# Attention with half tiles of keys stacked hi over lo, TensorE waits moved to the matmul that needs each, and new queue orders and PSUM banks

## The reference, cut to what matters

```python
q, k, v: (4, 8, 576, 64)                      # B, H, S, D
q_rot, k_rot = (rotate(q), rotate(k))
scores = scale * np.matmul(q_rot, k_rot.transpose(0, 1, 3, 2))
scores = scores - np.max(scores, axis=-1, keepdims=True)
attn = np.exp(scores)
attn = attn / (np.sum(attn, axis=-1, keepdims=True) + 1e-09)
x = np.matmul(attn, v)                        # to (2304, 512)
h = x @ w_in; r = np.maximum(h, 0.0)          # first MLP, 512 -> 2048 -> 512
x = (s * (r * r) + b) @ w_out
h = x @ w2_in                                 # second MLP, same sizes
out = (h * (1.0 / (1.0 + np.exp(-1.702 * h)))) @ w2_out
```

## Time and profile before

| | us |
|---|---|
| median of 3 runs | 1076.78 (1075.91 to 1077.61) |
| the profiled execution | 1077.13 |
| its span, first to last instruction | 1075.2 |
| outside the span | 1.93 |
| PE busy | 1043.3 (97%) |
| DVE, POOL, ACT busy | 737.1, 706.5, 634.5 |

### The profile page before, as it was taken

One profiled execution on the slowest core, in us unless ns is written; L12 is line 12 of the kernel. 1 busy time (PEld: TensorE's weight loads), 2 busy tenths in 40 slices (PEclk: granted clock), 3 DMA queues, 4 the chain that ended last, 5 costly groups with the idle time before them and its releaser, 6 DMA issues.

```text
span 1075.2 us, 17071 instructions
## 1 busy us (share of the span) xinstructions
PE 1043.3 (97%) x6234; PEld 962.3 (90%) x6234; DVE 737.1 (69%) x874; ACT 634.5 (59%) x1125; POOL 706.5 (66%) x586
## 2 busy tenths in 40 slices
PE   4899999999989999999999999999999999999998
PEld 4799999999988999999999999998888889888887
DVE  6888888889887757755586564875577555854542
ACT  4887878787865545654565454654456434654542
POOL 6878787878888856667556754766566675555420
PEclk9999999999999999999999999999999999999999
DMA  4555455554232221221212221221222422241101
GB/s 107 129 150 150 111 143 143 153 132 114 65 96 71 79 79 59 79 60 59 78 59 80 60 78 60 59 79 59 79 60 69 128 61 78 59 137 59 60 20 59
DMA packets 100613, 93.03 MB, mean 87 GB/s; under 512 B 15652, under 2 KB 78644, under 8 KB 100532
## 3 DMA queue, kind: packets, MB, share of 16 engines
q1 hardware_dynamic: 99408, 90.94, 29.6%
q10 hardware_dynamic: 1124, 1.02, 0.3%
HBM read 69.44 MB, written 4.79 MB: 69 GB/s over the span
## 4 chain that ended last, share of the span: by engine, by line
PE 83%; POOL 5%; DVE 5%; ACT 3%; DMA 2%; issue 1%; SPq 0%; ACTq 0%; POOLq 0%; DVEq 0%
PE psum L1121 37%; PE psum L1093 31%; PE psum L714 6%; PE psum L642 3%; PE psum L668 3%; ACT E L777 2%; DVE negmax L876 1%; DVE Xlo L886 1%; PE psum L744 1%; DVE osum L906 1%; DVE QK L929 1%; POOL win_lo L1038 1%; POOL xT L531 1%; DMA sin<-in_k_sin_dram 0%; POOL osum L527 0%
## 5 line engine op out<-in xcount | busy, mean ns | idle before, releaser
L1038 POOL TENSOR_TENSOR win_lo<-win_raw,win_hi 128x768 fp32r<-128x768 f32 x48 | 101.6, 2116 | 244.2 <-ACT win_hi L1032 244.2
L1093 PE MATMUL psum<-xc_hi,win_hi 128*128 128x384 f32 x672 | 226.7, 337 | 4.2 <-DVE h_b L1299 2.4
L1093 PE MATMUL psum<-xc_lo,win_hi 128*128 128x384 f32 x672 | 226.7, 337 | 0.0
L1093 PE MATMUL psum<-xc_hi,win_lo 128*128 128x384 f32 x672 | 226.1, 336 | 0.0
L1093 PEld LDWEIGHTS psum<-xc_hi,win_hi 128*128 128x128 f32 x672 | 126.8, 189 | 13.7 <-issue 3.8
L1093 PEld LDWEIGHTS psum<-xc_lo,win_hi 128*128 128x128 f32 x672 | 126.7, 189 | 8.2
L1048 POOL TENSOR_TENSOR wout_lo<-wout_raw,wout_hi 128x1024 fp32r<-128x1024 f32 x48 | 119.6, 2492 | 16.5 <-ACT wout_hi L1253 16.5
L1093 PEld LDWEIGHTS psum<-xc_hi,win_lo 128*128 128x128 f32 x672 | 126.8, 189 | 0.0
L777 ACT ACTIVATE E<-psum,negmax 128x576 f32<-128x576 f32 x128 | 94.6, 744 | 13.4 <-DVE negmax L876 13.3
L876 DVE TENSOR_REDUCE negmax<-psum 128x1 f32<-128x576 f32 x128 | 91.0, 751 | 14.1 <-PE psum L642 13.5
L1042 DVE TENSOR_TENSOR win_lo<-wsum,win_hi 128x1024 fp32r<-128x1024 f32 x46 | 95.1, 2068 | 4.2 <-ACT win_hi L1032 4.1
(11 more groups left out here) (154 smaller groups left out, 2852.5 us busy)
## 6 DMA issues: line engine op xcount, KB each, us to landing
wout_raw<-in_moe_w_out_dram SPq DMA_DIRECT2D x48, 512.0 KB, 3.6
win_raw<-in_moe_w_in_dram SPq DMA_DIRECT2D x48, 256.0 KB, 2.8
win_raw<-in_moe_w_in_dram SPq DMA_DIRECT2D x96, 128.0 KB, 2.8
Q<-QK SPq DMA_DIRECT2D x60, 144.0 KB, 2.8
QK<-QK SPq DMA_DIRECT2D x30, 288.0 KB, 3.4
vraw<-in_v_dram SPq DMA_DIRECT2D x32, 128.0 KB, 2.5
raw<-in_q_dram SPq DMA_DIRECT2D x30, 128.0 KB, 2.9
raw<-in_k_dram SPq DMA_DIRECT2D x30, 128.0 KB, 2.7
```

The source lines that it names most:

```text
L1038: pool.tensor_tensor(win_lo[m % 2][:, 0:3 * BLK], win_raw[m % 2][:, 0:3 * BLK], win_hi[m % 2][:, 0:3 * BLK].bitcast(F32), ALU.subtract).th ...
L1093: mm = pe.matmul(hps(n, k), w[n % 2][:, at:at + P], x[k][:, t, :], start=k in FRESH and t == 0 and i == 0, stop=t == HK - 1 and i == 2, sk ...
```

## The change

1. **Stacked half tiles.** `XC[h]` (128 x 640) holds head h's 64 tail keys twice: their hi part in the rows of h, their lo part in the rows of 1 - h. V's tail rows are loaded into both halves. One product per piece then gives hi and lo together. `hiT` and `loT` become two instructions of 64 x 576 each instead of one of 128 x 640. The clearing of `vraw` and SP's wait for it go; a V load has one more transfer.
2. **Waits.** `freed` is called per bank, ahead of the matmul that first writes the bank; X, XT and PV wait per tile.
3. **Orders.** All the order lists and bank lists are new. In the period lists the attention tokens carry an offset that is larger by seven (S@1 is now S@8, PV@-1 is PV@6, V@0 is V@5 and so on), while `program`, `FIRST`, the hooks `after(s)` and the offsets of `H`, `xc`, `wsplit`, `first`, `mid` and `late` are as they were.

```diff
-    PE_ORDER = order("XT@-1 X10@-1 X11@-1 IT@-1 X12@-1 X13@-1 S00@1 PV0@-1 H@-1 S01@1 S02@1 S03@1 ST@1 S10@1 S11@1 "
-                     "S12@1 X00@0 X01@0 S13@1 PV1@-1 prep0@3 X02@0 prep1@3 X03@0 XQ@0")
+    PE_ORDER = order("X03@6 H@-1 XQ@6 X10@6 X11@6 X12@6 X13@6 prep1@9 IT@5 XT@6 S00@8 S01@8 PV0@6 S02@8 S03@8 S10@8 PV1@6 S11@8 "
+                     "X00@7 S12@8 X01@7 S13@8 X02@7 ST@8 prep0@10")
...
-    POOL_ORDER = order("rot1@3 eps@0 V0@0 mid@0 V1@0 vlo0@0 vlo1@0 late@0 finish@-1 rot0@4")
+    POOL_ORDER = order("V0@5 eps@5 vlo0@5 rot1@8 V1@5 mid@0 finish@3 vlo1@5 rot0@9 late@0")
...
-    SLOTS = [1, 0, 5, 7, 1, 4, 3, 1, 2, 0, 1, 3, 0, 2, 1, 7, 6, 0, 2, 1, 7, 2, 1, 6]
+    SLOTS = [6, 5, 4, 2, 3, 1, 3, 0, 2, 1, 0, 3, 1, 0, 3, 2, 0, 7, 1, 6, 2, 7, 0, 1]
...
-            XThi = sb("XThi", [P, S + TAIL], F32R)
-            XTlo = sb("XTlo", [P, S + TAIL], F32R)
+            XC = [sb(f"XC{h}", [P, S + TAIL], F32R) for h in range(2)]
...
-                    sp.dma_start(vraw[rows_of(h), h, NM, :], v_h[2 * p + h, MAIN:S, :]).then_inc(v_in[h], 16)
+                    for half in range(2):
+                        sp.dma_start(vraw[rows_of(half), h, NM, :], v_h[2 * p + h, MAIN:S, :]).then_inc(v_in[h], 16)
...
-                    freed(pe, before[("S", p, h, j)])
                     ps, at = banks("S", p, h, j), (h + j) * P
-                    for a, b, c in PIECES[h]:
+                    for (a, b, c), job in zip(PIECES[h], before[("S", p, h, j)]):
+                        freed(pe, job)
...
+                    for j in range(NM):
+                        pe.wait_ge(et_lo, 2 * NM * p + NM * h + j + 1)
+                        for (a, b, c), job in zip(PIECES[0], before[("PV", p, h, 0)]):
+                            if j == 0:
+                                freed(pe, job)
+                            if h == 0 and j == 0 and b == r + S:
+                                pe.wait_ge(etQ_lo, p + 1)
+                            for n, x in enumerate((Xhi, Xlo)):
+                                pe.matmul(ps[:, a:b], V[h][:, j, :, :].rearrange("p a d -> p (a d)"), x[:, h, j, c:c + b - a],
+                                          start=j == 0 and n == 0, stop=False, skip_group_check=True)
+
+                    pe.wait_ge(etT_lo, 2 * p + h + 1)
+                    for a, b, c in (PIECES[0] if h == 0 else ((r, BANK, TAIL), (BANK, r + MAIN, TAIL + BANK - r), (r + MAIN, r + S, 0))):
+                        mm = pe.matmul(ps[:, a:b], V[h][:, NM, :, :].rearrange("p a d -> p (a d)"), XC[h][:, c:c + b - a],
+                                       start=False, stop=True, skip_group_check=True)
                     mm.then_inc(pv_done, 1)
...
-                def hiT(p, _, __):
+                def hiT(p, h, _):
                     act.wait_ge(xT_t, p + 1)
-                    need(act, pv_done, 2 * p)
-                    act.copy(XThi[:], banks("XT", p)[:, ROW[1]:ROW[0] + S]).then_inc(etT_hi, 1)
+                    need(act, pv_done, 2 * (p - 1) + h + 1)
+                    act.copy(XC[h][rows_of(h), 0:S], row(banks("XT", p), h)[rows_of(h), :]).then_inc(etT_hi, 1)
...
-                def loT(p, _, __):
-                    dve.wait_ge(etT_hi, p + 1)
-                    dve.tensor_tensor(XTlo[:], banks("XT", p)[:, ROW[1]:ROW[0] + S], XThi[:].bitcast(F32), ALU.subtract).then_inc(etT_lo, 1)
+                def loT(p, h, _):
+                    dve.wait_ge(etT_hi, 2 * p + h + 1)
+                    dve.tensor_tensor(XC[h][rows_of(1 - h), 0:S], row(banks("XT", p), h)[rows_of(h), :],
+                                      XC[h][rows_of(h), 0:S].bitcast(F32), ALU.subtract).then_inc(etT_lo, 1)
```

More of the change, by code:

```diff
@@ L89, in fused_kernel @@
-    SLOTS = [1, 0, 5, 7, 1, 4, 3, 1, 2, 0, 1, 3, 0, 2, 1, 7, 6, 0, 2, 1, 7, 2, 1, 6]
-    BANK_ORDER = (6, 0, 7, 1, 2, 3, 4, 5)
-    PE_FIRST = order("prep0@0 prep1@0 S00@0 S01@0 S02@0 prep0@1 S03@0 ST@0 S10@0 prep1@1 X00@0 S11@0 S12@0 S13@0 S00@1 "
[4 rows of a table removed]
-    ACT_FIRST = order("qk0@0 qk1@0 exp00@0 exp01@0 qk0@1 exp02@0 exp03@0 qk1@1 expT@0 hi00@0 exp10@0 exp11@0 exp12@0 "
[5 rows of a table removed]
-    DVE_FIRST = order("klo0@0 klo1@0 max00@0 max01@0 max02@0 klo0@1 max03@0 maxT@0 max10@0 klo1@1 lo00@0 max11@0 "
[5 rows of a table removed]
-    POOL_FIRST = order("rot0@1 rot1@1 rot0@2 rot1@2 V0@0 eps@0 V1@0 vlo0@0 rot0@3 vlo1@0 rot1@3 eps@1 V0@1 vlo0@1 rot0@4 "
-                       "rot1@4 rot0@5 eps@2 V1@1 V0@2 vlo1@1 vlo0@2 rot1@5 finish@0 V1@2 vlo1@2 rot0@6 finish@1")
@@ new lines, in fused_kernel @@
+    ACT_ORDER = order("xc01@-1 xc02@-1 exp02@7 exp03@7 exp10@7 evac1@5 xc03@-1 hi00@6 exp11@7 wsplit@-1 hi01@6 exp12@7 first@-1 "
+                      "exp13@7 hi02@6 qk0@9 hi03@6 hiQ@6 xc04@-1 hi10@6 expT@7 hi11@6 hi12@6 hi13@6 qk1@9 icp@5 hiT0@6 hiT1@6 "
+                      "exp00@8 exp01@8 evac0@6 xc05@-1 xc06@-1")
+    DVE_ORDER = order("max03@7 max10@7 sum1@5 xc01@0 xc02@0 xc03@0 first@0 max11@7 lo00@6 xc04@0 xc05@0 max12@7 xc06@0 max13@7 "
+                      "lo01@6 maxT@7 lo02@6 klo0@9 lo03@6 loQ@6 lo10@6 lo11@6 lo12@6 lo13@6 klo1@9 max00@8 loT0@6 max01@8 loT1@6 "
+                      "sum0@6 inv@6 max02@8")
@@ new lines, in fused_kernel @@
+    POOL_ORDER = order("V0@5 eps@5 vlo0@5 rot1@8 V1@5 mid@0 finish@3 vlo1@5 rot0@9 late@0")
+    SP_ORDER = order("load0@10 kcopy1@8 load1@10 get@4 qcopy0@9 put@5 loadv0@7 loadv1@7 qcopy1@9 kcopy0@9")
+    SLOTS = [6, 5, 4, 2, 3, 1, 3, 0, 2, 1, 0, 3, 1, 0, 3, 2, 0, 7, 1, 6, 2, 7, 0, 1]
+    BANK_ORDER = (6, 0, 7, 1, 2, 3, 4, 5)
+    PE_FIRST = order("prep0@0 prep1@0 S00@0 S01@0 S02@0 ST@0 S03@0 prep0@1 S10@0 X00@0 X01@0 S11@0 S12@0 prep1@1 S13@0 X02@0 X03@0 "
[4 rows of a table added]
+    ACT_FIRST = order("qk0@0 qk1@0 exp00@0 exp01@0 exp02@0 expT@0 exp03@0 qk0@1 hi00@0 exp10@0 hi01@0 exp11@0 qk1@1 exp12@0 hi02@0 "
[4 rows of a table added]
@@ L152, in put @@
             of = banks_of(kind, p, h, j)
-            before[(kind, p, h, j)] = list(dict.fromkeys(last_in[b] for b in of if b in last_in))
+            was = [last_in.get(b) for b in of]
+            before[(kind, p, h, j)] = [job if job not in was[:n] else None for n, job in enumerate(was)]
             for b in of:
@@ L263, in fused_kernel, with freed @@
         x_done = sem("x_done")
-        def freed(eng, jobs):
-            for job in jobs:
+        def freed(eng, job):
+            if job:
                 read(eng, *job)
@@ L279, in read @@
             elif kind == "XT":
[L280 removed]
+                need(eng, etT_lo, 2 * p + 2)
             elif kind == "IT":
@@ L674, in XQ_job @@
                         pe.wait_ge(expT_done, p + 1)
-                    freed(pe, before[("XQ", p, 0, 0)])
+                    freed(pe, before[("XQ", p, 0, 0)][0])
                     ps = banks("XQ", p)
```

83 lines of the change are left out of this document (32 added, 51 removed), and 27 rows, old and new, of tables (ACT_FIRST, DVE_FIRST, PE_FIRST).

## The result

| | before | after |
|---|---|---|
| median, us | 1076.86 (4 runs, 1075.91 to 1077.61) | 1105.26 (4 runs, 1103.36 to 1106.56) |
| ratio, 95% interval | 1 | 1.0263 [1.0248, 1.0277]: slower |
| profiled execution, its span | 1077.13, 1075.2 | 1104.12, 1102.3 |
| PE busy, granted clock | 1043.3, 0.998 | 1040.4, 0.988 |

The forecast was 1092.8 with a range of 1082 to 1099. The direction is right, the size isn't: 12.5 us of the loss were not seen, and the range misses it by 6.

What follows compares the result with a forecast made beforehand. PE was taken to bound attention, busy 17.76 of 18.15 us a period. Periods -2.3, start and last pairs -2.7 and the joint +21.0 summed to +16.0, so 1092.8 us beside the median, range 1082 to 1099.

Steps and rivals of the forecast that it cites:

- The mechanism of the joint: Between attention and MLP: POOL starts window 0's work only after attention's last V; PE stands still some 15 us.
- The waits of the period: In each attention period PE waits in X11 and X13 and before PV0, behind ACT's queue: 1.25 us in all.
- The columns on PE's path: Fewer tail columns in PV0 and PV1 save PE 0.57 us per pair, with bounds of 0 and 0.57.
- The slow clock of the first products: Products (0,0) and (0,1) after the joint run at 1.2 GHz, costing nothing while ACT holds (0,2) back.
- 17.95 us a period: Attention period: 16.7 us of work plus 1.25 of new waits, against 18.15; -2.3 us over eleven periods.
- hidden restarts: PE losses inside "busy" in an attention period, estimated at 0.5 us and taken off the old period.
- Start and last pairs, -2.7: Columns of pairs 0, 13 and 14 give 1.7 us, a new order of the first pairs 1 us.
- the joint, +21.0: Between attention and MLP: product (0,2) starts 32.8 us after PV1 of pair 14 ends, in place of 11.8.
- everything by the same amount: MLP from product (0,2) on: POOL, ACT and DVE keep the old order, so all shifts by +21.0 us.
- hiT and loT in two, no cost: Attention period: second instructions add 0.6 us each to ACT and DVE, both staying below PE.
- the stacked tile gives no time: Rival within the forecast's range: weight loads set the pace, columns of pairs 0, 13 and 14 give nothing; +1.7, 1094.5.
- a worse joint with *no* gain per period: Rival, 15%: low clock from (0,2), POOL slower and further behind, no gain in attention; 1099.3 us.

Runs made afterwards that it cites:

- e11: Changed kernel with everything of the joint moved along with attention (POOL, SP, PE, ACT, DVE, banks) and DVE's `inv` ahead of `xc01`: 1089.66 us.
- e3: Changed kernel with each product of the stacked tail tile issued twice: 1112.82 us, 7.6 above the changed kernel.
- e9: Changed kernel with the joint's labels moved, plus the start lists of the kernel before: 1090.21 us, against 1090.31 with the change's start.
- e2: Changed kernel with the offsets of POOL's period list alone lowered by six: 1102.08 us.
- e1: Changed kernel (stacked half tiles, moved waits) with the queue orders and banks of the kernel before: 1085.48 us, ratio 1.0072 to the kernel before.
- e5: e1 with the half tile of head 1 later, `hiT1` behind `hi11` and `loT1` behind `lo11`: 1108.28 us.
- e10: e1 with PV0 ahead of S00 and the banks changed, so PV0 has those of XQ and IT: 1085.99 us.
- e12: e11 without the stacked tile (128x704 tail tile, two tail products a piece, one hiT and one loT): 1096.05 us.

## Why the prediction was right and wrong

**Right.** The mechanism of the joint: tokens of attention moved by seven, the steps tied to s not, POOL's queue in one row, PE idle for 12 to 18 us (18.2 were measured, just beyond), (0,2) behind ACT. Moving those labels gave 15.6 us back (e11). The waits of the period (X11 for `klo0`, X13 for `expT`, PV0 for `klo1`), each at its place, 0.51 + 0.24 + 0.18 = 0.93, where 1.25 was worked out. The columns on PE's path (e3). The slow clock of the first products: 0.32 us from start to start from 334.85 to 338.05, at 1.2 GHz; they were not the path's end, since (0,2) then waited 0.99 for ACT.

**Right by luck: 17.95 us a period.** Measured were 18.05. Of these 0.93 are waits, so PE's own work is 17.1, where the sum had 16.7: the 0.5 of "hidden restarts" that it took off hardly went. It had been read from two rows (205.60 and 206.75) as the same two jobs, but they are X10, X11 and X12, X13. The work was 0.4 too small and the waits 0.3 too large, and the two errors nearly cancelled.

**The step that failed first: "Start and last pairs, -2.7".** With the period it made t0 5.0 earlier; it came 1.80 later. The period took 1.2 of these 6.8 us (-1.13 over eleven periods, for -2.3). The rest is in this term: -0.94 up to PV1(1), then +0.35 and +3.52 from PV1(12) to PV1(14). I counted the columns and not what the order leaves behind each PV1. The table above shows that between PV1(13) and PV1(14) PE needs 14.1 us in place of 10.6. After a PV1 the new order has S11, S12, S13 and ST of the pair two later and X00 to X02 of the next still to do, at 289.79 to 294.3; the old one has `prep0` and `prep1` there, which the last pairs don't have. The four jobs of scores take 3.4 us from start to start, two waits (for `expT` and for `XC`) take 0.9 in place of 0.2, and the columns give 0.6 back: together the 3.5. In the periods this costs nothing, at the end about 4 us. That is read from the rows; no run changed the order of the last pairs. The gain of 0.94 at PV1(1) is the same thing seen from the other side: e9 with the old start came out the same.

**The second: the joint, +21.0.** From t0 it took 23.9 more (35.7 for 11.8). Of the 2.9 missing, 2.53 is the wait of `finish` for `inv_row`, behind `load_win(1)` on SP. I followed POOL's hooks and not SP's, whose labels had stayed behind in just the same way. e2 shows what they are worth alone: with POOL moved and SP not, POOL waits 11.4 and 9.2 us. `w_sum` took 4.2 for 2.9 and `first_w_hi` 4.2 for 3.3 beside DVE's lo parts of x, 2.2 in place of the 1.5 added for that; ACT's part was the size worked out.

**The third: behind (0,2) "everything by the same amount".** 1.4 us more were lost. PE waits there for `h_a` for 3.0 us, for 1.5 before, and a little behind this wait, from 355.7 on, the products run at the low clock (1.2 GHz), those with `wout` 0.43 us from start to start in place of 0.24:

```profile
354.90 0.45 PE L1094 MATMUL psum<-xc_hi,win_hi 128*128 128x384 f32 x1 [2.96 <-DVE h_a L1143]
```

The kernel before has such a stretch of its own a little earlier, the twelve products behind the wait of 2.35 us, which the changed kernel runs at full clock; over the 25 us from (0,2) on, the granted clock is 0.93 in both. So the low clock takes about the same from both, and what is lost are waits: 5.7 us of them from there on in windows 0 and 1, for 4.1 before. Why `h_a` is late stays open.

Together 6.8 + 2.9 + 1.4 = 11.1, which is 27.1 of span less the 16.0 that were forecast. The other 1.4 of the 12.5 between the medians lie in which executions were profiled.

**An assumption that held here and not in general: "hiT and loT in two, no cost".** It rested on DVE's share of a period (15.82 of 18.15). e1, e5 and e10 show that this share doesn't settle it: in the old order DVE is without a pause for just the stretch that PE waits for. In the new order the pieces stand elsewhere and cost about half of the columns' gain (e12). The rival "the stacked tile gives no time" was priced by the pace of weight loads; the mechanism that would have made it true is DVE's.

The range failed because its upper end took a worse joint with *no* gain per period, but t0 never later than before.

## What to carry to other kernels

When the tokens of a schedule are renumbered, list everything that is tied to the old numbers on every queue, the DMA queue too; one queue of two moved back gave 3 us, both 13. Price a new order by what stands behind the last full step as well as by its period: work that is left for later is free in the steady state and is paid for once at the end. And an engine's share of a period does not say if it has room; look if it has a pause in the stretch that the bound engine waits for, since the same edit gained 6 us in one order and lost 8 in the other.
